# Adding the experts' results to the tokens' rows in place

## The reference

```python
    do_compute = skip_score > 0
    xc = x[do_compute]
    e_idx = np.argmax(logits, axis=1)
    gate_w = probs[np.arange(len(xc)), e_idx]
    for e in range(E):
        h = np.maximum(xc[mask] @ w1[e], 0.0)
        y[mask] = gate_w[mask, None] * (h @ w2[e])
    out[do_compute] = xc + y
...
    h = x @ w_in
    g = np.maximum(0.01 * h, h)
    return (g @ w_out)
```

## Time and profile before

| | us |
|---|---|
| runs, lowest / median / highest (3) | 773.31 / 775.59 / 780.62 |
| the profiled execution | 770.11 |
| its span, first to last instruction | 768.4 |
| PE busy in the span | 722.8 (94%) |

### The profile page before, as it was taken

One profiled execution on the slowest core, in us unless ns is written; L12 is line 12 of the kernel. 1 busy time (PEld: TensorE's weight loads), 2 busy tenths in 40 slices (PEclk: granted clock), 3 DMA queues, 4 the chain that ended last, 5 costly groups with the idle time before them and its releaser, 6 DMA issues.

```text
span 768.4 us, 12937 instructions
## 1 busy us (share of the span) xinstructions
PE 722.8 (94%) x4664; PEld 672.0 (87%) x4664; DVE 275.3 (36%) x589; ACT 242.0 (32%) x522; POOL 185.3 (24%) x190
## 2 busy tenths in 40 slices
PE   4999979894989999998999999999999999999997
PEld 3898879883989999997989999989998999899986
DVE  5757747657100000003332243233223323332222
ACT  3467656451111111123222322222222232223222
POOL 3120100102588777543000400130031004001000
PEclk9999989895899999999999999999999999999999
DMA  8473745772699999983000200030021003001001
GB/s 188 120 182 94 183 128 167 248 256 70 217 279 334 335 335 358 337 243 85 17 1 1 96 29 1 28 96 1 0 77 46 0 12 111 0 0 42 1 1 41
DMA packets 72441, 91.47 MB, mean 119 GB/s; under 512 B 26872, under 2 KB 47896, under 8 KB 72401
## 3 DMA queue, kind: packets, MB, share of 16 engines
q1 hardware_dynamic: 62289, 62.70, 27.7%
q0 software_dynamic: 9056, 28.23, 11.8%
q10 hardware_dynamic: 1056, 0.02, 0.1%
HBM read 73.91 MB, written 17.01 MB: 118 GB/s over the span
## 4 chain that ended last, share of the span: by engine, by line
PE 80%; SPq 10%; DMA 4%; issue 2%; DVE 2%; POOL 1%; ACT 1%; ACTq 0%; POOLq 0%; DVEq 0%
PE psum L1654 26%; PE psum L1673 26%; PE psum L1556 9%; PE psum L1572 8%; SPq L429 6%; SPq L424 2%; PE psum L1396 2%; DMA x_rows<-xo 2%; PE psum L1421 1%; PE psum L1512 1%; PE psum L1495 1%; SPq L414 1%; PE psum L1636 1%; DMA xg<-x_rows,idx 1%; PE psum L1582 1%
## 5 line engine op out<-in xcount | busy, mean ns | idle before, releaser
L1654 PE MATMUL psum<-x2h,wih 128*128 128x384 f32 x384 | 130.6, 340 | 1.9 <-DVE x2l L1316 1.9
L1334 DVE SCALAR_TENSOR_TENSOR g_act<-g_raw 128x384 f32<-128x384 f32 x96 | 53.6, 558 | 219.1 <-ACT g_raw L995 218.7
L1654 PE MATMUL psum<-x2h,wil 128*128 128x384 f32 x384 | 129.4, 337 | 0.0
L1654 PE MATMUL psum<-x2l,wih 128*128 128x384 f32 x384 | 128.9, 336 | 0.0
L995 ACT ACTIVATE g_raw<-psum 128x384 f32<-128x384 f32 x96 | 47.1, 491 | 235.0 <-PE psum L1654 235.0
L1673 PE MATMUL psum<-woh,g_l 128*128 128x512 f32 x288 | 114.0, 396 | 0.0
L1673 PE MATMUL psum<-wol,g_h 128*128 128x512 f32 x288 | 113.8, 395 | 0.0
L1673 PE MATMUL psum<-woh,g_h 128*128 128x512 f32 x288 | 112.2, 389 | 0.7 <-DVE g_l L1338 0.7
L1556 PE MATMUL psum<-xt,wring 128*128 128x160 f32 x512 | 82.6, 309 | 0.6 <-issue 0.6
L792 POOL DMA_INDIRECT out_dram<-o_sb,idxo x15 | 15.9, 1060 | 277.3 <-ACT o_sb L990 274.3
L1572 PE MATMUL psum<-hp,wring 128*128 128x160 f32 x512 | 78.5, 302 | 0.0
(11 more groups left out here) (197 smaller groups left out, 892.1 us busy)
## 6 DMA issues: line engine op xcount, KB each, us to landing
wring<-in_moe_w_dram SPq DMA_DIRECT2D x64, 512.0 KB, 9.8
q_st<-in_q_dram SPq DMA_DIRECT2D x8, 576.0 KB
k_st<-in_k_dram SPq DMA_DIRECT2D x8, 576.0 KB
x_sb<-x_rows SPq DMA_DIRECT2D x4, 1024.0 KB, 6.2
stage<-in_moe_w_in_dram POOLq DMA_DIRECT2D x4, 1024.0 KB, 10.1
stage<-in_moe_w_out_dram POOLq DMA_DIRECT2D x4, 1024.0 KB, 11.1
y_rows<-zrow POOLq DMA_DIRECT2D x7, 480.0 KB, 6.9
vs<-in_v_dram SPq DMA_DIRECT2D x20, 128.0 KB, 6.9
```

Source lines behind the costliest of these rows:

```text
L1334: dve.scalar_tensor_tensor(out=g_act[:, f % 2, :], in0=g_raw[:, f % 2, :], scalar=LEAK, in1=g_raw[:, f % 2, :], op0=ALU.mult, op1=ALU.max) ...
L1654: last = pe.matmul(bank[f % 2][:, 0:MT * P], wt[:, c, f * P:(f + 1) * P], xp[:, T.par, c, :], start=(c == 0 and n == 0), stop=(c == KD - 1 ...
```

## The change

The result of a tile is no longer stored as a row of y. DVE adds it to the gathered row at once, `yr = psum * gate + xg`, reading PSUM directly, and POOL scatters `yr` back into `x_rows` with an indirect DMA. For this

- the gate is needed per slot: three bf16 parts of it go through 18 more matmuls next to those of the overflow index (moved from f = 5 to f = 8 of tile 0), and DVE adds them up; it also makes `tok_put` (where to scatter; empty slots go to spare rows behind the tokens) and `tok_get` (empty slots read a row of zeros);
- `xg` has two buffers; from tile 1 on `x_turn` stands at f = 6, and it is left out in tile 7;
- POOL's round i >= 1 waits for `s_x2r` (DVE has added tile i-1), gathers tile i+1, scatters tile i-1 and, at the end of the round, waits for that scatter and then frees `yr` (`put_done`, semaphore `s_yf`);
- the zero fill of `y_rows`, the stores of y, the gathers of y and DVE's `x2_rows` in the last network are gone; the rows `x3` of the first 384 are gathered in round 7, ahead of its `stage_split`.

```diff
-            y_rows(T.i0 + (T.d - 1))
-            x_copy(T.i0 + (T.d + 1), 1 - par)
+            x2_rows(T.i0 + (T.d - 1), 1 - par)
+            if ahead:
+                x_copy(T.i0 + (T.d + 1), 1 - par)
...
+            def x2_rows(i, par, at_=2):
+                dve.wait_ge(s_yt, i * 2 + 2)
+                if isinstance(i, int) and i == 0:
+                    dve.wait_ge(s_tok_o, 2)
+                dve.tensor_copy(gate2[:, :], gate_s[:, 2 * i:2 * i + 2] if isinstance(i, int)
+                                else gate_s[:, bass.ds(i * 2, 2)]).then_inc(s_g2, 1)
+                dve.wait_ge(s_g2, i + 1)
+                dve.wait_ge(s_yf, i + 1)
+                for hf in range(2):
...
+                    dve.scalar_tensor_tensor(out=yr[:, hf, :], in0=bank[at_ + hf][0:HALF, :],
+                                             scalar=gate2[:, hf:hf + 1], in1=x_, op0=ALU.mult,
+                                             op1=ALU.add).then_inc(s_x2r, 1)
...
             for i in range(2 * NU):
-                pool.wait_ge(s_xt, 2 * (i + 1))
-                gather_x(i + 1)
+                if i == 0:
+                    pool.wait_ge(s_xt, 2)
+                    gather_x(1, 1)
+                else:
+                    if i == 1:
+                        pool.wait_ge(s_zd, 16)
+                    pool.wait_ge(s_x2r, 2 * i)
+                    if i + 1 < E:
+                        gather_x(i + 1, (i + 1) % 2)
+                    put_x(i - 1)
...
                 if i == 0:
-                    pool.wait_ge(s_tok_o, 1)
+                    pool.wait_ge(s_tok_o, 2)
+                if i == 2 * NU - 1:
+                    pool.wait_ge(s_srt, 16)
+                    indices(0)
+                    gather_rows(s_gm)
                 stage_split(i)
...
+                if i:
+                    put_done(i - 1)
...
                     if f == 1 and not first:
+                        pe.wait_ge(s_tok_o, 2)
                         y_turn(T.i0 + (T.d - 1))
...
-                    if f == 3:
+                    if ahead and f == (3 if first else 6):
                         if not first:
-                            pe.wait_ge(s_tok_o, 1)
-                        for hf in range(2):
-                            pe.wait_ge(s_xf[hf], 1 if first else T.n(2, 1))
-                        x_turn(T.i0 + (T.d + 1))
-                    if first and f == 5:
+                            pe.wait_ge(s_x2r, T.n(2, 0))
+                        x_turn(T.i0 + (T.d + 1), 1 - par)
+                    if first and f == 8:
```

More of the change, by code:

```diff
@@ L755, in _ @@
             pool.wait_ge(s_plan, 2)
+            pool.wait_ge(s_zd, 16)
             tiles = pool.value_load(plan[0:1, 31:32], min_val=E, max_val=TILES)
[L757 to L772, removed]
+            last_tile = pool.value_load(plan[0:1, 30:31], min_val=E - 1, max_val=TILES - 1)
+            with pool.If(tiles > E):
+                gather_x(E, 0)
+                with pool.Fori(0, NOV // 2) as i2:
+                    for u in range(2):
+                        i = i2 * 2 + (E + u)
+                        with pool.If(i < tiles):
+                            pool.wait_ge(s_x2r, i * 2)
+                            carry()
+                            gather_x(i + 1, 1 - u)
+                            put_x(i - 1)
+                            put_done(i - 1)
+                        with pool.Else():
+                            pass
+                pool.wait_ge(s_x2r, tiles * 2)
@@ L783, in scatter_out @@
+                gather_rows(s_gr)
+                for j in range(MT):
+                    pool.wait_ge(s_gr[j], 16)
+                pool.sem_inc(s_rd, 1)
+            with pool.Else():
+                pool.sem_inc(s_rd, 1)
+                pool.wait_ge(s_x2r, 2 * E)
+                put_x(E - 1)
+                put_done(E - 1)
             def scatter_out(m):
-                pool.tensor_copy(idxo[:, :], column(m * MT, 0)).then_inc(s_io, 1)
+                pool.tensor_copy(idxo[:, :], column(m * MT)).then_inc(s_io, 1)
@@ L942, in tile @@
                                    ).then_inc(s_hp, 1)
-                    if f == 4:
+                    if ahead and f == (4 if first else 6):
                         x_copy(T.i0 + (T.d + 1), 1 - par)
-                    if f == 1 and not first:
-                        y_rows(T.i0 + (T.d - 1))
                 act.wait_ge(s_l2, T.n(FC, FC))
@@ L1341, in mstep @@
                         outputs(T)
-                    if not last and f == 5:
-                        x2_rows(T.i0 + (T.d + 1))
                     if not last and f in (8, 10, 12):
@@ L1616, in _ @@
                     tile(Tile(i2 * 2, u + 1))
-            tile(Tile(0, E - 1))
+            tile(Tile(0, E - 1), False)
             with pe.If(tiles > E):
+                for hf in range(2):
+                    pe.wait_ge(s_xf[hf], E)
+                pe.wait_ge(s_x2r, 2 * (E - 1))
+                x_turn(E, 0)
                 with pe.Fori(0, (NOV + 3) // 4) as i4:
```

334 lines of the change are left out of this document (169 added, 165 removed).

## The result

| | before | changed kernel |
|---|---|---|
| runs | 4 | 4 |
| lowest / median / highest, us | 773.31 / 775.35 / 780.62 | 793.55 / 802.20 / 815.55 |
| ratio, 95% interval | | 1.0298 [1.019, 1.0407] |
| profiled execution, us | 770.11 | 815.55 |
| its span, us | 768.4 | 813.8 |

The change makes the kernel 3.0% slower, about 23 us by the ratio; 772.3 us within 768 to 777 was forecast. The ratio leaves out the profiled execution of the changed kernel, which is 2.8% above the fastest of its four runs at a lower mean clock (0.953 against 0.965 to 0.970) and whose span grew by 45 us; so the places are read from it, and the size from the ratio.

The account below looks back on a forecast made before the run. PE was taken as the bound, with 80% of the chain of waits. Tile 0 +1.08, tile 1 -4.27 and the step to the last network -0.1 sum to -3.3 us: 772.3 us, range 768 to 777.

Parts of the forecast that it names:

- rival 2: Tiles 2 to 6: POOL's round is longer than a tile, giving 781 to 790 us; chance 0.06.
- Off PE: Work on DVE, ACT, POOL and DMAs lies beside a busy PE, so removing or adding it counts 0.
- Tile 0, +1.08: Tile 0: 18 new gate matmuls hold PE 1.08 us, so tile 1 starts that much later.
- Tile 1, -4.27: Tile 1: PE's gap at x_turn and the low clock behind it vanish, giving back 4.27 us.
- the landing taken at 4.4: Tile 1: the gather of tile 2 lands 4.4 us after its start, so PE has no gap.
- Rival 1: Tile 1: gather of tile 2 is late all the same; 773.5 to 776 us if the clock falls; chance 0.28.
- Tiles 2 to 6, 0: POOL's ring of 17.9 us keeps up with a tile of 18.87, so no gap and 0 change.
- Tile 7 to the last network, -0.1: The 0.56 us saved by leaving out x_turn is eaten by DVE; last network starts after 24.4 instead of 24.52.
- Attention is untouched: Attention gets only one small DMA on ACT's queue, before a wait for weights; counted as 0.
- as unchanged: Last network: PE runs without gaps and keeps 12 transposes for each step, so no change.
- Rival 4: Larger saving: gates cost 0.68, last network starts 1 us earlier: 771 us; an edge of the forecast's 0.62.
- rival 3: POOL's end or DVE's order delays the last network 1 to 2 us: 773.5 us; an edge of the forecast's 0.62.

Follow-up runs that it names:

- e1: Changed kernel with sort records of 16 bytes again instead of 4: 772.92 us against 771.05 for the kernel before, ratio 1.0036.
- e11: The kernel of e1 run again, on one chip with e12: 774.04 us against 769.48 for the kernel before, ratio 1.0067.
- e6: e1 with the index and gate matmuls of tile 0 back at f = 5: 768.67 us against 771.18 for the kernel before, 0.9977.
- e12: e6 plus DVE making x2l before adding the last tile's rows, on one chip with e11: 767.60 us against 769.48 for the kernel before, 0.9968.
- e5: e1 with DVE's copy of the two gates made by a one-element reduction: 769.29 us against 771.18 for the kernel before, 0.9978.
- e10: The kernel of e12 plus the gate copy made by a reduction as in e5: 772.08 us against 772.24 for the kernel before, 0.9999.
- e4: Kernel before with 18 more scatters of 4-byte records to a tensor nobody reads: 814.72 us against 771.05, ratio 1.0547.
- e8: Control of e4: kernel before with the same 18 extra scatters, but of 16 bytes: 773.44 us against 771.18, ratio 1.0022.
- e2: Changed kernel with 4-byte sort records placed 64 bytes apart: 772.04 us against 771.05 for the kernel before, ratio 1.0014.

## Why the prediction was wrong

**The step that failed.** It is the sentence under rival 2 on the five indirect DMAs that hold POOL, "three scatters of tiny rows, so what they move seems not to matter", together with "Off PE". For POOL it was right: an indirect DMA holds it about 1.0 us, with 4 bytes or 2 KB. But the prediction asked of the records only how long they hold POOL. What they do to the DMA engines was priced nowhere, though the order rows showed `2304x4` becoming `2304x1`, and though it stated that the DMAs are at 1.0 of their capacity. An edit that seemed to make a transfer smaller got no line in the sum. It is worth some 18 to 20 us, by the ratios 1.0298 with it and 1.0036 (e1) and 1.0067 (e11) without. None of the four rivals had it; it fell into the 0.04 for anything else.

**The forecast's own terms**, read in e1, where the records are repaired:

- Tile 0, +1.08: right. +1.0 in e1; in the changed kernel the 36 matmuls hold PE from 209.13 to 210.91 (the start of tile 1 less a share), 1.78 with 1.76 forecast.
- Tile 1, -4.27: wrong, by 4.8; it became +0.5. Two of its steps failed. The first is "DVE has added tile 0 (`y_turn` ends at 213.32 + 3.2 = 216.5, two additions to 218.3), so this is not what is late": the small copy ahead of the additions had been given no time, and took 4.07 behind POOL's split, which the sentences just before had moved to that place. The second is the landing taken at 4.4: it was 5.3 in e1, 5.6 in e6, e11 and e12, and 6.7 in e5, each above the 5.1 that the prediction named as its sign. The row of before at this very place said 6.7; the prediction put that down to the zero fill, and without the fill the landing is 1.4 us shorter at best, not 2.3. Rival 1 is what happened: by its numbers tile 1 would have come to between -1.0 and 0.0 with the clock (-4.27, plus 1 or 2 of gap, plus 2.24), and it came to +0.5, by a cause that it did not have.
- Tiles 2 to 6, 0: right, once the records are repaired: 94.30 us in e1 against 94.31 before (235.38 to 329.69), with the round of POOL at 16.0 (223.45 to 239.46). Rival 2 did not occur.
- Tile 7 to the last network, -0.1: 24.27 in e1 (24.4 forecast, 24.52 before), 24.71 in the changed kernel. There PE, DVE and PE again show:

```profile
393.86 1.04 PE L1614 MATMUL psum<-ident,yt 128*80 128x128 f32 x8 [1.54 <-issue]
...
398.60 0.44 PE L1694 MATMUL psum<-x2h,wih 128*128 128x384 f32 x1 [2.39 <-DVE x2l L1350]
```

```profile
395.35 1.41 DVE L1310 SCALAR_TENSOR_TENSOR yr<-psum,gate,xg 80x512 f32<-80x512 f32 x2
396.67 1.87 DVE L1350 TENSOR_TENSOR x2l<-psum,x2h 128x512 fp32r<-128x512 f32 x3
```

  `x2l` stands right behind the addition, as the prediction said. With the order turned (e12), the last network starts 23.86 after tile 7's start. The term was right.
- "Attention is untouched", and the last network, taken "as unchanged": +0.4 and +1.1 in e1. The second is the clock. In e1 PE is idle for 1.10 and 2.39 us at this step and then runs at 0.50 from 357.3 to 360.9, a price of 1.7 us; before (1.23 and 1.91 idle) and in e12 (1.35 and 1.74) the clock stays at 1.00 there, and the last network of e12 is within 0.2 of before. So DVE's addition ahead of `x2l` did cost, though not in the term that had it. The +0.4 I can't place.

So the intended gain exists in part: with the records as they were, the index back at `f == 5` and `x2l` first, the forecast of -3.3 us comes out at about -2 (medians -1.8 and -1.9, ratios 0.9974 and 0.9968, on two chips); with the reduction added, on a third chip, it did not show (e10). In the trace of e12 tile 1 gives back 4.07 of the 4.27, tile 0 costs 0.56, and the stretch ahead of it, which the forecast had at 0, is 1.4 us longer than before; whether that is the change or the chip no run shows. Rival 4 did not show, and of rival 3 only the clock behind DVE's order.

## What to carry to other kernels

Price every edit of a transfer on the engine that carries it, not only on the one that issues it; a table row whose shape changes, even to something smaller, gets its own line. Where DMA engines are near a busy share of 1.0 and something waits for a stream, look at busy share and GB/s together in windows of 2 to 10 us: full share with a quarter of the rate is work that the byte count doesn't show. And before a small DVE operation is put on a path, see what POOL runs at that moment.

## What the runs showed of the hardware

- Indirect scatters of 128 records of 4 bytes that lie next to each other brought the DMA engines to 24 to 74 GB/s at a busy share of 0.65 to 1.06 for some ten microseconds; three in each of six rounds cost some 18 to 20 us (changed kernel) and 44 (e4). The same with 16 bytes cost 2 us (e8, 1.0022 [0.9998, 1.0046]), 4 bytes at a pitch of 64 nothing that was measured (e2, [0.9996, 1.0032]), and 8, 16 and 64 bytes side by side raised no wait for the weights, though with 8 the engines moved 47 GB/s at 0.93 for 6 us.
- The Trainium skill (DMA: Bandwidth & Descriptors, "Specifications") says that a transfer of less than 512 bytes makes the DMA engine read, modify and write. By that rule alone 4, 16 and 64 bytes would be alike; the runs show that they are not, so how close the records lie matters too. By what mechanism no run here shows; two writes to the same 64 bytes waiting for each other would fit e2, but in e1 four records share them and nothing waits.
- A DVE copy of 160 values took 4.07 us under a POOL operation that had begun 0.5 us ahead of it, and ended with it; a reduction over the same values took 0.15 under the same POOL operation (e5), and behind it, still under that operation, the two additions that read PSUM and SBUF took 0.70 each.
- A gather of 80 rows of 2 KB took 4.9 to 6.7 us to land beside the weights' stream (tiles 1 to 6 in e1, e5 and e12), and 6.6 to 7.8 in the kernel before, which has a large fill ahead of it.
- PE's clock stood at 0.50 for 3.6 us behind idle rows of 1.10 and 2.39 us (e1), and stayed at 1.00 behind 1.35 and 1.74 (e12) and behind a single row of 0.63 (e5).
